# A mixture-of-experts kernel: the second expert's weight load moved behind the third step's rows

## What is computed

```python
def _moe2_ref(x, w_gate, w_output_gate, w1, w2):
    logits = x @ w_gate                       # (4608, 8)
    e_idx = np.argmax(logits, axis=1)
    ...
    for e in range(E):
        mask = e_idx == e
        if not mask.any():
            continue
        h = np.maximum(x[mask] @ w1[e], 0.0)  # w1[e]: 512 x 1024
        ye = h @ w2[e]                        # w2[e]: 1024 x 512
        out[mask] = gate_w[mask, None] * eom[mask, e, None] * ye
```

## Time and profile before

| What | Value |
|---|---|
| median of 3 runs | 1140.67 us (1140.27 to 1140.86) |
| the profiled execution | 1143.34 us, with a span of 1141.7 us from its first to its last instruction |
| mean granted TensorE clock | 0.993 |
| PE busy | 1108.4 us, 97% of the span |
| DVE, ACT, POOL busy | 623.4, 402.0 and 206.9 us |
| DMA traffic | 149.81 MB, mean 131 GB/s |
| the second expert's load | 4 x 512 KB and 2 x 1024 KB, issued from 725.71 us on |

### The profile page before, as it was taken

How to read it: one execution, slowest core, us unless ns; L and a number is a source line. 1 busy time by engine, 2 the same in 40 slices (tenths; PEclk the granted TensorE clock), 3 DMA queues, 4 the chain that set the end, 5 groups by cost and what they waited for, 6 DMA issues and landing times.

```text
span 1141.7 us, 18312 instructions
## 1 busy us (share of the span) xinstructions
PE 1108.4 (97%) x6514; PEld 897.7 (79%) x6515; DVE 623.4 (55%) x1365; ACT 402.0 (35%) x752; POOL 206.9 (18%) x298
## 2 busy tenths in 40 slices
PE   5999999999999999999999999999999999989995
PEld 2777777777777777777777889889998989878884
DVE  6584484664754854845745566573333336366332
ACT  3444334334434433343343355141121124244211
POOL 1000011020020020110200303432232233333321
PEclk8999999999999999999999999999999999999998
DMA  9398197495692891920130301691111124453120
GB/s 337 108 288 255 53 290 219 120 294 148 185 301 76 249 294 45 307 81 1 38 74 26 104 1 39 175 255 37 55 55 37 55 56 98 151 114 113 39 55 20
DMA packets 73002, 149.81 MB, mean 131 GB/s; under 512 B 11231, under 2 KB 12511, under 8 KB 72928
## 3 DMA queue, kind: packets, MB, share of 16 engines
q1 hardware_dynamic: 59696, 115.34, 35.7%
q0 software_dynamic: 13248, 33.71, 10.0%
HBM read 131.11 MB, written 92.01 MB: 195 GB/s over the span
## 4 chain that ended last, share of the span: by engine, by line
PE 87%; DVE 7%; issue 2%; DMA 2%; ACT 1%; DVEq 0%; another core or an unknown queue 0%; POOLq 0%; POOL 0%; SPq 0%; ACTq 0%
PE bank L501 27%; PE bank L503 26%; PE bank L502 26%; PE bank L534 2%; PE bank L552 1%; PE bank L568 1%; DMA s_in<-rows_dram 1%; PE bank L576 1%; DVE g_buf L1174 1%; PE bank L512 1%; DVE w_lo L1311 1%; DMA XT<-xT_in_dram 1%; PE bank L541 0%; DVE gT_lo L1178 0%; DVE v_lo L1156 0%
## 5 line engine op out<-in xcount | busy, mean ns | idle before, releaser
L501 PE MATMUL bank<-wout_lo,gT_hi 128*128 128x512 f32 x544 | 216.1, 397 | 0.0
L503 PE MATMUL bank<-wout_hi,gT_hi 128*128 128x512 f32 x544 | 212.5, 391 | 0.0
L502 PE MATMUL bank<-wout_hi,gT_lo 128*128 128x512 f32 x544 | 212.3, 390 | 0.0
L1174 DVE TENSOR_TENSOR g_buf<-g_buf,bank 128x512 f32<-128x512 f32 (+1 forms) x144 | 94.3, 655 | 104.1 <-ACT g_buf L927 104.1
L501 PE MATMUL bank<-xgT_lo,w_hi 128*128 128x256 f32 x512 | 145.3, 284 | 2.6 <-DVE w_lo L1311 2.6
L503 PE MATMUL bank<-xgT_hi,w_hi 128*128 128x256 f32 x512 | 144.5, 282 | 0.0
L502 PE MATMUL bank<-xgT_hi,w_lo 128*128 128x256 f32 x512 | 144.5, 282 | 0.0
L927 ACT ACTIVATE g_buf<-bank 128x512 f32<-128x512 f32 (+1 forms) x144 | 82.5, 573 | 149.8 <-PE bank L503 148.4
L1178 DVE TENSOR_TENSOR gT_lo<-g_buf,gT_hi 128x512 fp32r<-128x512 f32 (+1 forms) x144 | 95.4, 662 | 72.9 <-ACT gT_hi L933 70.7
L933 ACT CAST gT_hi<-g_buf 128x512 fp32r<-128x512 f32 (+1 forms) x144 | 85.9, 597 | 136.4 <-DVE g_buf L1174 133.9
L403 POOL DMA_INDIRECT rows_dram<-y_buf,row_i x34 | 35.4, 1040 | 542.3 <-DVE row_i L1268 534.7
(11 more groups left out here) (218 smaller groups left out, 1745.1 us busy)
## 6 DMA issues: line engine op xcount, KB each, us to landing
rows_dram<-x_in_dram SPq DMA_DIRECT2D x17, 4128.0 KB
xq<-rows_dram POOLq DMA_DIRECT2D x88, 128.0 KB, 2.9
raw<-w_dram SPq DMA_DIRECT2D x20, 512.0 KB
raw<-w_dram SPq DMA_DIRECT2D x10, 1024.0 KB, 11.3
X<-x_in_dram SPq DMA_DIRECT2D x8, 1024.0 KB
XT<-xT_in_dram SPq DMA_DIRECT2D x7, 1024.0 KB, 5.6
win<-w_in_dram SPq DMA_DIRECT2D x4, 1024.0 KB, 13.4
y_buf<-w_out_dram POOLq DMA_DIRECT2D x6, 512.0 KB, 6.0
```

The source lines that it names most:

```text
L501: pe.matmul(o, l_hi, r_lo, start=first, stop=False)
L502: pe.matmul(o, l_lo, r_hi, start=False, stop=False)
L503: return pe.matmul(o, l_hi, r_hi, start=False, stop=last)
L1174: dve.tensor_tensor(g_buf[:, n, 0:w], g_buf[:, n, 0:w], up_b[n][:, 0:w], ALU.max).then_inc(g_ready, 1)
```

## The change

The wait of SP ahead of its first `load_planned` asks for 240 in place of 160 on `rows_in`: the second expert's weights are requested once the third step's rows have landed, and no longer once the second step's have.

```diff
             sp.wait_ge(ctl_ready, 1)
-            sp.wait_ge(rows_in, 160)
+            sp.wait_ge(rows_in, 240)
 
             def load_planned(v):
```

## The result

| | before | after |
|---|---|---|
| median | 1140.76 us (4 runs) | 1148.86 us (4 runs) |
| ratio of the runs | | 1.0066, 95% interval 1.0054 to 1.0078 |
| profiled execution, span | 1143.34, 1141.7 us | 1148.69, 1147.1 us |
| mean granted clock | 0.993 | 0.991 |

The change makes the kernel 0.7% slower, by 7.5 us by the ratio and 8.1 by the medians; 1148.2 was forecast. The spans differ by only 5.4 us, since the two profiled executions differ ahead of the change too: ACT's first hT_hi of the second step starts at 728.13 before and at 725.22 after, 2.9 us earlier. From it to the first hT_hi of the fourth step, before takes 774.66 - 728.13 = 46.53 us and after 780.04 - 725.22 = 54.82: 8.29 more. From there to the end of the span it is 367.04 and 367.06 us, so nothing behind the fourth step's start adds to the loss.

A forecast was written before the change was run, and what follows sets the result against it. PE was taken to bound the kernel (busy 1108.4 of 1141.7 us). A new 7.9 us wait less 1.97 gained gives +5.9, plus 1.6 for the clock, +7.5 on 1140.67: 1148.2 us, range 1143.9 to 1151.2.

The forecast's parts named there:

- What bounds the kernel, and what the late rows cost: PE bounds the kernel; the third step's late rows cost it 1.97 us in the second step, which the change removes.
- The shift of SP's issue: SP's first issue of the second expert's weights moves from 725.71 to 734.5, later by 8.8 us.
- The transfer: The second expert's weight load takes 20.2 us, bounds 16.2 to 22.7, so w2 lands at 754.7, 6.2 us later.
- The string behind it: From w2's landing, ACT and DVE work in program order takes 7.9 us to the third step's first hT_hi.
- Net and clock: PE waits 7.9 us in the third step, less 1.97 gained, net +5.9; the lower clock adds 1.6.
- The clock's bound: Low clock on PE's work behind the wait: at most 4.6 us at half speed, so 2.3 us lost.
- Faster: Rival: w1 slow only from sharing, whole load at 399 GB/s, no new PE wait; 1138.7 us, chance 0.06.
- A second collision: Rival: third expert's w1 meets the end of the second's w2; +10.7 us, 1151.4; over 1151.2 has chance 0.03.
- The range's lower edge: 1144.2 us, lower end of the forecast case, for w2 landing 4 us late without the clock.

The follow-up runs named there:

- e7: Kernel before (wait for 160), with ACT and DVE steps written out and the second expert's weights split in the third step: 1141.77 us, ratio 1.0008.
- e6: Changed kernel (wait for 240), with ACT and DVE steps written out and the second expert's weights split in the third step: 1139.24 us, ratio 0.9982.
- e3: Kernel before (wait for 160), with w1 laid out so each DMA fills 128 partitions instead of 32: 1138.96 us, ratio 0.9972.
- e5: Changed kernel (wait for 240), with ACT and DVE's second and third steps written out, split still in the second: 1150.12 us, ratio 1.0079.
- e4: Kernel before, but only two of w1's four DMAs go ahead of the wait for 240, the rest and w2 behind it: 1147.62 us, ratio 1.0051.
- e2: Changed kernel (wait for 240), with w1 laid out so each DMA fills 128 partitions instead of 32: 1148.48 us, ratio 1.0054 against the kernel before.
- e8: Changed kernel, PE's second and third steps written out, the third's fourth hidden block made six times: 1153.8 us, ratio 1.0115 against the kernel before.
- e9: Changed kernel with PE's second and third steps written out and no block repeated: 1152.45 us, ratio 1.0084 against the kernel before.
- e10: Changed kernel, PE's second and third steps written out, the third's fourth hidden block made eight times: 1154.0 us, ratio 1.0092 against the kernel before.
- e11: Kernel before, with w1 over 128 partitions and SP's wait raised to 320, the fourth step's rows: one run, 1152.46 us.
- e1: Changed kernel with SP's wait raised from 240 to 320, the fourth step's rows: 1156.65 us, ratio 1.0132 against the kernel before.

## Why the prediction was right

- **What bounds the kernel, and what the late rows cost.** Right. The second step lost 1.97 us to them and no longer does; e7 against e6 shows it alone, at 2.3 us in the stretch (46.8 against 44.5).
- **The shift of SP's issue.** 8.8 us was forecast. Counted from the second step it is 732.65 - 725.22 = 7.43 against 725.71 - 728.13 = -2.42, so 9.85. Of the 1.05 too little, 0.5 is s_in's landing (3.0 us, where the median of 2.5 was taken and 3.1 stood as the bound), and 0.6 is SP's way from release to issue: 729.6 to 732.65 is 3.0 us, where 2.45 was read from before.
- **The transfer.** 20.2 forecast, 19.6 measured (732.65 to 752.29). So w2 is taken 6.8 us later, not 6.2.
- **The string behind it.** Right to the tenth: 752.29 + 7.9 = 760.2, where PE starts. Since PE comes to its fifth block 26.5 us after the second step's first hT_hi (22.28 - 1.42 + 4 x 1.42), its wait should be w2's time less 18.6. The table bears that out in seven kernels, from w2 at 23.9 to 34.1, within 0.1 us each; and e3, at 18.2, has none.
- **Net and clock.** PE waited 8.5 us, not 7.9, for a net of 6.5, not 5.9. The clock took 1.75 us where 1.6 was taken, and 6.5 + 1.75 = 8.3 is what the stretch shows. The mechanism was right; that the total came within 0.7 us of the forecast (1148.86 against 1148.2) is in part luck. The shift was 1.05 too small and the transfer 0.6 too long, which partly cancel. The clock's term was luck altogether: it was carried over from a low stretch behind a wait of 2.6 us, and that stretch was misread. By the half microseconds at 0.54 and 0.55 it runs from 1015.54 to 1018.95, 3.4 us, not 3.2. Behind the long waits of the table the low clock on work ranges from 2.9 to 6.0 us, and e5 has 4.4 of it behind nearly the same wait.
- **The clock's bound** was wrong in general: at most 2.3 us, I wrote. e4's took 3.0 and e2's 2.7, behind shorter waits. The waits of 2.6 us for w_lo and of 5.3 us and more for hT_lo were all followed by work at half clock. The length of a wait alone doesn't decide it, for e8's of 3.1 us at 1009 left the clock at full. But e9 and e10 show that in the third step the idling is the cause. The Trainium skill (TensorE: Matmul & The Clock Gate, "HAM oscillation — how this bites in real kernels") says that after a long enough wait for a transfer the work starts again at the lower clock; the waits of the table, 5.3 to 15.5 us, agree.
- **The rivals.** "Faster" needed a landing at 746.8 on the clock of before, a transfer of 12.3 us. Even w1 over 128 partitions with nothing beside it took 13.2 (e11). Its reason was wrong as well: w1 is slow by its shape and not by what it shares, for with nothing beside it the load takes 17.8 us in e1's shape and 13.2 in e11's. Only its last step holds, that with w2 in time just the gain is left: e3's stretch has neither wait. That e3's 1138.96 is near the rival's 1138.7 says little, as its gain is to be read against the runs of the kernel before on that chip, whose median is 1142.3: by the ratio it is 3.2 us, not 2.0. The Trainium skill (DMA: Bandwidth & Descriptors, "Rules for kernel authors") asks for 128 partitions for full bandwidth; e11 against e1 agrees. "A second collision" didn't happen: the third expert's w1 does go out at 752.16 in the changed kernel, at the end of w2, but from the fourth step's start to the end before and after agree within 0.02 us.
- **The range's lower edge.** A landing 4 us late gives 1140.67 + 4 - 0.3 = 1144.4, not 1144.2; nothing hangs on it.

## What to carry to other kernels

A transfer that is in the way of a small one may itself have no slack: before moving it back, look at how long the engine that takes it had waited, and follow what that engine does next in program order, here 7.9 us of it to an engine that is full. The wait that goes (2 us) is then replaced by a longer one (8.5 us). The net loss is the delay of the landing less the slack (6.8 - 0.3 = 6.5 us), plus the clock. Two edits kept the gain without the loss. One leaves the early issue alone and makes the transfer shorter: w1's wider shape in e3 (ratio 0.9972). The other keeps the late issue and moves the use a step later: e6 (ratio 0.9982). The later use alone, with the early issue, gains nothing (e7, 1.0008).

## What the runs showed of the hardware

- How long the clock stays low on the work behind a wait isn't set by the wait: 3.5 us behind 8.5, 2.9 behind 15.5, 5.4 behind 6.0, 6.0 behind 5.3. The clock fell 2.5 (e5) to 5.2 us (the change) into the long waits of the table. In e4 and e2 that was only 0.8 and 1.4 us before PE took up work, so most of the low stretch lay on work; in e1 it was 10.8 us before. What sets the moment of the fall isn't shown. A wait of 5.3 or 6.0 us cost half as much again by it.
- 512 KB transfers into 32 partitions each ran at 195 to 262 GB/s, the same bytes over 128 partitions at 373 to 410 (e1 and e11, without rows under way).
- The 512 KB of a step's rows add 1.8 us to a 4.19 MB load that is half made of 32-partition transfers, and 4.1 us to one that isn't: the rate is 219 to 275 GB/s while they pass, against some 390 without them.
- An interrupted load (e4: two DMAs, a wait for rows, four DMAs) took 26.5 us in all, against 22.7 for the load of before, which went out in one piece beside the rows.
